# Linear attention and two MLP blocks on one core: the order of work at the start of the first unit, the waits of the middle row and statistics, and one store

## The reference

```python
# linear attention with a decay per channel
for t in range(S):
    state = alpha[:, :, t, :, None] * state + np.einsum('bhd,bhe->bhde', k[:, :, t], v[:, :, t])
    y[:, :, t] = np.einsum('bhd,bhde->bhe', q[:, :, t], state)
x = y as (B, S, H * D) = (4, 768, 384)
# first block
xn = (x - mu) / np.sqrt(var + 1e-06) * g_ln
x = x + np.maximum(xn @ w_ch1, 0.0) @ w_ch2
# second block
u = x + np.real(np.fft.fft(np.fft.fft(x, axis=1), axis=2))
un = (u - mu) / np.sqrt(var + 1e-06)
out = u + np.maximum(un @ w2_ch1, 0.0) @ w2_ch2
```

## Time and profile before

| what | value |
|---|---|
| median of 3 runs | 809.58 us (809.53 to 810.5) |
| the profiled execution | 808.13 us, its span 806.6 us |
| TensorE matmul (PE) busy | 791.1 us, 98% of the span |
| VectorE (DVE) busy | 460.6 us, 57% |
| ScalarE (ACT) busy | 239.2 us, 30% |
| GpSimd (POOL) busy | 77.3 us, 10% |
| mean granted TensorE clock | 0.998 |

### The profile page before, as it was taken

The page is one execution under the profiler, slowest core; times in us unless marked ns, Lnnn a source line. Parts: engine busy times, 40 slices in busy tenths (PEclk is TensorE's granted clock), DMA queues, the critical chain, the costliest instruction groups (busy, mean ns, idle before and its releaser), DMA issues.

```text
span 806.6 us, 13042 instructions
## 1 busy us (share of the span) xinstructions
PE 791.1 (98%) x4934; PEld 780.5 (97%) x4934; DVE 460.6 (57%) x1011; ACT 239.2 (30%) x450; POOL 77.3 (10%) x119
## 2 busy tenths in 40 slices
PE   6899999999999999999999999999999999999998
PEld 5799999999999999999999999999999999999998
DVE  7895765746747647476577685345643464342322
ACT  4434332232332412422434432212221222121211
POOL 2335000000000000000000400120002000210000
PEclk9999999999999999999999999999999999999999
DMA  9624213131032051323304431120000200000000
GB/s 199 154 79 128 61 33 81 35 89 31 29 88 59 3 131 52 90 64 103 128 1 145 140 112 51 54 98 31 1 30 22 104 2 0 29 0 30 1 30 30
DMA packets 60299, 51.37 MB, mean 64 GB/s; under 512 B 26460, under 2 KB 59996, under 8 KB 60252
## 3 DMA queue, kind: packets, MB, share of 16 engines
q1 hardware_dynamic: 60252, 50.74, 23.0%
HBM read 41.29 MB, written 13.37 MB: 68 GB/s over the span
## 4 chain that ended last, share of the span: by engine, by line
PE 85%; DVE 7%; DMA 5%; SPq 1%; POOL 1%; issue 1%; ACT 0%; DVEq 0%; POOLq 0%; ACTq 0%
PE h L44 11%; PE acc L46 11%; PE acc L44 11%; PE acc L45 11%; PE h L46 11%; PE h L45 11%; PE side_bank L1301 5%; PE side_bank L1265 5%; DMA x_turned<-x_scratch 4%; PE side_bank L1297 2%; PE side_bank L1309 2%; PE side_bank L1278 1%; SPq L478 1%; PE side_bank L45 1%; PE side_bank L46 1%; PE side_bank L44 1%
## 5 line engine op out<-in xcount | busy, mean ns | idle before, releaser
L121 DVE SCALAR_TENSOR_TENSOR hT_low<-h,hT_high 128x384 fp32r<-128x384 f32 x192 | 106.5, 555 | 191.7 <-ACT hT_high L116 191.5
L44 PE MATMUL h<-xnT_high,w_high 128*128 128x384 f32 x576 | 205.6, 357 | 2.6 <-DVE hT_low L121 2.3
L116 ACT ACTIVATE hT_high<-h 128x384 fp32r<-128x384 f32 x192 | 94.3, 491 | 349.7 <-PE h L46 349.7
L46 PE MATMUL h<-xnT_high,w_low 128*128 128x384 f32 x576 | 194.2, 337 | 0.0
L45 PE MATMUL h<-xnT_low,w_high 128*128 128x384 f32 x576 | 194.0, 337 | 0.0
L44 PE MATMUL acc<-w_high,hT_high 128*128 128x384 f32 x576 | 193.9, 337 | 0.0
L46 PE MATMUL acc<-w_high,hT_low 128*128 128x384 f32 x576 | 192.8, 335 | 0.0
L45 PE MATMUL acc<-w_low,hT_high 128*128 128x384 f32 x576 | 192.6, 334 | 0.0
L44 PEld LDWEIGHTS h<-xnT_high,w_high 128*128 128x128 f32 x576 | 108.8, 189 | 4.3 <-issue 2.9
L45 PEld LDWEIGHTS h<-xnT_low,w_high 128*128 128x128 f32 x576 | 108.9, 189 | 1.1
L46 PEld LDWEIGHTS h<-xnT_high,w_low 128*128 128x128 f32 x576 | 108.5, 188 | 0.0
(11 more groups left out here) (118 smaller groups left out, 836.6 us busy)
## 6 DMA issues: line engine op xcount, KB each, us to landing
stage<-w_dram SPq DMA_DIRECT2D x24, 384.0 KB, 3.2
v_pad<-v_dram SPq DMA_DIRECT2D x16, 288.0 KB, 5.2
x_scratch<-x_unit SPq DMA_DIRECT2D x8, 576.0 KB, 3.0
a_in<-alpha_dram SPq DMA_DIRECT2D x7, 576.0 KB, 4.9
q_in<-q_dram SPq DMA_DIRECT2D x7, 576.0 KB, 7.0
k_in<-k_dram SPq DMA_DIRECT2D x7, 576.0 KB, 8.7
xb<-x_scratch SPq DMA_DIRECT2D x4, 576.0 KB, 4.2
xb<-x_turned SPq DMA_DIRECT2D x4, 576.0 KB, 6.6
```

The source lines that it names most:

```text
L44: pe.matmul(out, wh, xh, start=start, stop=False)
L46: return pe.matmul(out, wl, xh, start=False, stop=stop)
L116: act.activation(self.hT[0][:, j % H_SLOTS, :], self.hps[j % H_BANKS][:, 0:UN], ACT.Relu).then_inc(self.h_high, 1)
L121: dve.scalar_tensor_tensor(out=self.hT[1][:, j % H_SLOTS, :], in0=self.hps[j % H_BANKS][:, 0:UN], scalar=0.0, in1=self.hT[0][:, j % H_SLOT ...
```

## The change

Five edits, in four places:

- ScalarE: `spread_q(1, 0)` moves from ahead of unit 0's first relu to behind its second.
- VectorE: ahead of unit 0 only `scan_forward(1, 0)` is left; `scale_q(1, 0)` comes behind the first `dve_low`.
- Weight pieces 3 and 4: their `low` moves from GpSimd to VectorE, at tiles 1 and 2 of unit 0; GpSimd goes on with piece 5 when they are done.
- `add_mid` waits for the first of GpSimd's three blocks and no longer for all; in exchange the statistics wait for each block.
- SyncE: the wait for the turning copy stands behind the store of `u_front` and no longer ahead of the loop.

```diff
-            sp.wait_ge(turned[1], 48)
             with sp.Fori(0, B - 2) as b:
                 store(b, 0, u_front)
+                sp.wait_ge(turned[1], 48)
                 sp.wait_ge(cos_read, UT * (b + 2))
...
             pool.wait_ge(xn_ready, UT)
-            for n in ONE_W[2:]:
+            split.low(pool, ONE_W[2])
+            pool.wait_ge(split.low_done, ONE_W[4] + 1)
+            for n in ONE_W[5:]:
                 split.low(pool, n)
...
                 high_xT(0, 0, k, g_col[:, k:k + 1])
-            spread_q(1, 0)
...
             def side_zero(j):
+                if j == 1:
+                    spread_q(1, 0)
                 for slot in DELAYED.get(j, (j,)):
...
                 dve.wait_ge(mid_summed, n + 1)
-                dve.wait_ge(u_ready, UT * n + UT)
+                dve.wait_ge(u_ready, UT * n + 1)
...
-            def norm_two(u, half, slot):
+            def norm_two(u, half, slot, n):
                 rows = (u_front, u_mirror)[half]
                 if slot == 7:
                     for i in range(UT):
+                        dve.wait_ge(u_ready, UT * n + i + 1)
                         statistics(NU + u, i, rows)
...
                 low_xT(0, 0, k, g_col[:, k:k + 1])
-            prepare_q(1, 0)
+            scan_forward(1, 0)
...
             def side_zero(j):
                 if j == 0:
+                    scale_q(1, 0)
                     prepare_k(1, 1, 0)
                 if j == 1:
+                    dve.wait_ge(split.low_done, ONE_W[2] + 1)
+                    split.low(dve, ONE_W[3])
                     side_one(0, 1, 0)
+                if j == 2:
+                    split.low(dve, ONE_W[4])
                 for slot in DELAYED.get(j, (j,)):
                     side_one(0, 1, slot)
```

More of the change, by code:

```diff
@@ L1199, in _ @@
                 if j in (9, 10):
-                    norm_two(0, 0, j - 2)
+                    norm_two(0, 0, j - 2, 0)
                 if j == 11:
-                    norm_two(0, 0, 10)
-                    norm_two(0, 0, 11)
+                    norm_two(0, 0, 10, 0)
+                    norm_two(0, 0, 11, 0)
                 if j > 1:
@@ L1220, in unit_two @@
                     if not (half == 1 and last):
-                        norm_two(u + 1, 1 - half, j)
+                        norm_two(u + 1, 1 - half, j, b + half)
                     if also:
```

## The result

The changed kernel takes 801.9 us (median of 4 runs, 801.9 to 803.35) against 809.56 of the kernel before (4 runs beside it, 809.42 to 810.5): ratio 0.9907, 95% interval 0.989 to 0.9925. That is 7.7 us less. The prediction was 803.9, 5.7 less, with a range down to 803.0: the direction was right, the gain too small, and the time is outside the range. The two profiled executions, 808.13 and 801.90, lie only 6.2 us apart (spans 806.6 and 800.4). So two things have to be explained: 0.5 us between 5.7 and 6.2, and 1.5 us between 6.2 and 7.7. Beside the 808.52 the changed kernel took 801.94, which is 6.6 us less.

What follows compares the result with a forecast made beforehand. TensorE was taken as the bound, busy 791.1 of 806.6 us. Gains of 4.6 (first unit), 0.6 (middle row) and 0.5 (store) sum to 5.7, so 809.58 becomes 803.9 us, range 803.0 to 806.3 for 8 in 10.

Steps and rivals of the forecast that it cites:

- The step that failed: Whole kernel: the median stays 1.45 us above the profiled execution, so 809.58 - 5.7 = 803.9 us.
- The clock as a term of the sum: First unit, from 39.40: the 3.55 us half-clock stretch goes with the hole before tile 2, worth 1.62 us.
- part A: First unit: reordered relu, spreading and weight pieces bring the second scores from 50.18 to 45.6, gaining 4.6 us.
- the decomposition 2.28 + 1.62 + 0.89: First unit's upper bound, 4.8 us: hole before tile 2, half-clock stretch, and second hole at `k_div` with its change-over.
- half clock anyway: Rival, first unit: the clock falls because of the whole start-up, not the 2.11 us hole; costs 1.62, giving 805.5; chance 0.10.
- cover for `k_div` of chunk 1: After the second scores: `k_div` comes at about 51.8, its transposes are asked for at 52.3; cover 0.5 us, the thinnest place.
- rival of VectorE as the bound: First unit: two pieces and GpSimd's blocking push `k_div` of chunk 1 or a mask past TensorE; 805.3 or 807.1; chance 0.17.
- B: Middle row and statistics: `add_mid` needing only the first block closes TensorE's hole near 462.3; gain 0.6 us, bounds 0 and 0.6.
- C: Store of `u_front` issued ahead of the copy's wait closes TensorE's hole near 518.2; gain 0.5 us, bounds 0 and 0.5.
- The queue rule: DMA queue: engines take descriptors in ring order, so the store's last share waits behind the copy; at hardest 0.5 us less gain.

Runs made afterwards that it cites:

- e13: The kernel before, unchanged, profiled once more: 809.71 us, with the second scores at 51.81.
- e14: The kernel before, unchanged, profiled once more: 808.02 us, with the second scores at 50.18.
- e3: Against the kernel before, only the relu ahead of the spreading and scale_q behind dve_low; weight pieces 3 and 4 stay on GpSimd: 808.49 us, ratio 0.9987.
- e4: Against the kernel before, only weight pieces 3 and 4 moved to VectorE; spread_q stays ahead of the first relu: 806.54 us, ratio 0.9962.
- e1: Against the kernel before, all edits of the first unit alone; middle row, statistics and store as before: 804.25 us, ratio 0.9935.
- e12: Changed kernel with 18 warming matmuls, but the store again behind the wait for the turning copy: 802.36 us, ratio to the kernel before 0.9907.
- e2: Against the kernel before, only middle row, statistics and store changed; first unit as before: 807.94 us, ratio 0.9989.
- e7: The kernel before with 8 dummy matmuls put into TensorE's hole before tile 2: 810.24 us against 808.52, ratio 1.0017.
- e9: The changed kernel with 18 instead of 14 warming matmuls at the start: 801.89 us, ratio to the kernel before 0.9915.
- e11: Changed kernel with 18 warming matmuls, but middle row and statistics as in the kernel before: 802.70 us, ratio to the kernel before 0.9911.
- e10: The kernel before with 18 instead of 14 warming matmuls at the start: 807.45 to 810.88 us, ratio 1.0.

## Why the prediction was wrong, point by point

**The step that failed** is the last one: "The median of the runs is 1.45 above the profiled one, so 809.58 - 5.7 = 803.9." I carried the 1.45 over as if it were a constant. e13 and e14 show what it is in the main: a stretch at 1.2 GHz that in some executions, the profiled one among them, fell where TensorE would have waited for `k_div` anyway, and in the others fell behind 45.07, where it costs 1.6. The change removes both holes, and no trace of the changed first unit (six of them) shows the stretch behind 33.92. From the kind of execution that the profile showed, the gain is 6.2; from the other kind it is 6.2 + 1.6 = 7.8, and by their times the four runs of before were of that kind, or had the stretch at the start besides. Of the 2.0 us between 803.9 and 801.9 this step has 1.45 and the sizes of the terms 0.5 (5.7 against 6.2). None of my rivals let the 1.45 go, so the lower end of the range, 803.0, had no case under it.

Part of the 1.45 was the draw. All three runs behind 809.58 were at 809.53 or above. Of the 51 later runs of the same kernel 25 are below 809, 14 between 809.05 and 809.81 and 12 above 810.5. A median of three can fall into any of these groups.

**The clock as a term of the sum.** I credited 1.62 us to the end of the half-clock stretch at 39.40. In the profiled execution it was nearly worthless: e13 has the full clock there and the transposes at 45.09 all the same. My total for part A held only because I had computed both ends of the path and taken their difference; the decomposition 2.28 + 1.62 + 0.89 named the wrong payer. `k_div` set 45.07. Each half of the edit brings its transposes forward by a part: the relu alone by 1.9 (e3, 45.07 to 43.16), the pieces alone by 2.5 (e4, 43.99 less the 1.40), both together by 4.8 (40.28). In the medians of whole runs they are worth 0.6, 2.5 and 4.8 us (e3, e4, e1); the relu alone keeps so little because it leaves a hole of 2.74 us, and in its trace the clock falls behind that. The rival "half clock anyway" priced the same 1.62 before `k_div`; the danger and the gain were in the stretch after it.

**Part A** otherwise went as computed: 4.72 measured, 4.6 predicted. `hT_low` at 36.30, `k_div` ended at 40.04 (40.2 predicted), second scores at 45.46 (45.6). GpSimd's pieces 5 and 6 did block VectorE from 44.88, but left 1.0 us of cover for `k_div` of chunk 1, where I had 0.5. The rival of VectorE as the bound is shown wrong by the trace.

**Parts B and C** were mis-sized terms: 0.6 and 0.5 predicted, and both called upper bounds. Taken back alone they measured 0.8 and 0.5. Between the two traces the queue's store of unit 7 moved by 5.49 (468.85 to 463.36), of which 4.67 had arrived at 417.50, so B is 0.8; the whole span moved by 6.2, which leaves 0.7 for C in that pair. The turning copy is not always ready equally soon: its last part, from issue to the store released by it, took 31.25 us before (483.24 to 514.49) and 31.26 in e12 (477.48 to 508.74), but the issue ahead of it took 10.56 and 10.25. So the hole that C closes differs from execution to execution: 0.50, 0.35, 0.32 and 0.21 in the traces of before, e14, e1 and e12.

Why a recorded hole is too small: a matmul of 384 columns is recorded for 0.34 us but steps on every 0.175, so the last record before a hole covers the first 0.17 of it. The weight loads come nearer: the hole recorded as 0.61 on TensorE before the transposes is 0.90 on PEld. For the hole before tile 2 I had added this 0.17; for B and C I had not. 4.72 + (0.61 + 0.17) + (0.50 + 0.17) = 6.17, against 6.2 measured.

**Rule against row.** The queue rule that the prediction cites did not make C worthless, but this case doesn't test it. The store landed at 510.0, 3.12 us after its issue, the same as in the earlier trace rows with the copy done (514.49 to 517.61). Its own data began to move only about 0.9 us after the issue, and by then the copy's were through:

```profile
507.60:507.80 0.20, 0.20 (x3) 1.00 0.14 54
507.80:508.00 0.20, 0.20 (x3) 1.00 0.93 338
```

The DMA share goes from the copy's 0.14 straight to the store's 0.93. In e12 the copy's share ends at about 508.0 as well, and the store that waits for it is issued at 508.74. So of the 1.86 us by which the store lands earlier (511.86 to 510.00) about 0.7 were the wait from the copy's last bytes to the issue, and 0.9 the store's own delay, which now passes while the copy still moves. The two transfers themselves hardly overlap.

**Open.** Which execution gets which stretch is not settled. Something differs between executions of one program already at the start: the 28 records of the 14 warming matmuls last 4.99 us in the first profile of the kernel before and 6.23 in e13. That this decides where the clock falls is not shown. The Trainium skill (TensorE: Matmul & The Clock Gate, "What's actually happening") says that throttling is the default and that recent activity lifts it. The traces agree in so far as every fall seen here began within 2 us of the end of a hole: of 1.59 us (e2), 1.99 (e7), 2.01 (e1) and 2.10 (e4) at the start, of 2.08 to 2.11 before tile 2, of 2.31 to 2.74 before `k_div`. But holes as long had no fall behind them: 2.44 (before) and 2.35 (e14) at the start, 2.10 before tile 2 in e4 and e13.

With 18 warming matmuls the hole at the start was 0.31 to 1.46 us in the four traces, with 14 it was 1.20 to 2.44 in ten. On the changed first unit 18 were seen in 13 runs (e9, e11, e12), all at a mean clock of 0.999 or 1.000; that is few to rule a fall out, and the 810.88 of e10 speaks for care.

## What to carry to other kernels

Before adding the distance between a profiled execution and the median to a forecast, ask what that distance is made of: if the mean clock of single runs differs, part of it may be a stretch at 1.2 GHz that the edit itself removes or exposes. Price a clock stretch only after asking what the engine would have done with the time; next to a wait for another engine it is free, a few microseconds later it costs 1.6. And read a hole on the row of the weight loads, or from start to start, since overlapping matmul records hide its first part.

A median of three runs of a program with several kinds of executions is a draw; here three came from the slower half. Ask how the runs are spread before a difference of 1.5 us is given a cause.

The version to keep is e9, the change with 18 warming matmuls: 801.89, the same as the changed kernel's best, but in each of its 5 runs.

## What the runs showed of the hardware

- The same program, with the same 2.1 us hole in TensorE's work, ran on at 2.4 GHz in e13 and fell to 1.2 GHz in the first profile, for 3.55 us; the fall of e13 came after its next hole, 2.31 us long, and lasted most of 3.9 us (mean clock 0.57).
- A stretch at 1.2 GHz of 7 us at the start (e4: mean clock 0.55 from 10 to 17) delayed the first unit by only 1.4 us. TensorE had idle time there to give: 2.38 of the 10.60 us from 9.40 to 20.00 in the first profile, 0.44 in e4. A shorter one in e2 (mean clock 0.53 from 10.4 to 14.0) delayed the transposes that stood at 17.57 by 0.36.
- Four more warming matmuls, run in the idle time before 9.4, cost nothing in four traces (e9 to e12): `k_div`'s transposes stayed at 9.42.
- A store of 576 KB moved its first data about 0.9 us after its issue and had landed 3.12 us after it, in the first profile, in e12 and in the changed kernel alike (e12: 508.74 to 511.86).
